# A fused attention and two-stage feed-forward kernel on one core: attention steps placed earlier in their slots, first moves joined, splits and last groups moved

## The chip, the cores and the metric

The kernel runs on one core of a Trainium2 chip. The metric is the device time of one execution in microseconds (us). Below, TensorE is the matrix engine (PE in the profile, PEld its weight loads), VectorE is DVE, the activation engine is ACT, GpSimd is POOL, and SyncE (SP) issues most of the DMAs. Each engine works through its own list of instructions in order and waits on semaphores that others raise.

## The reference

Three stages follow each other, all in float32.

```python
# 1. attention: B, H, S, D = 4, 8, 768, 48
for t in range(S):
    state = alpha[:, :, t, :, None] * state + einsum('bhd,bhe->bhde', k[:, :, t], v[:, :, t])
    y[:, :, t] = einsum('bhd,bhde->bhe', q[:, :, t], state)
# y becomes x of 3072 tokens by 384
# 2. four experts, each 384 -> 1024 -> 384
p = domain_probs / domain_probs.sum(-1)
out += p[:, e:e+1] * (maximum(x @ w1[e], 0) @ w2[e])
# 3. 384 -> 2048 -> 384
g = h - tanh(h)      # h = x @ w_in
result = g @ w_out
```

## The kernel before

Each float32 operand of a large product is kept as two rounded parts, a high one and the rest (low), and a product is three matmuls: high by high, high weights by low data, low weights by high data.

**Token sets and slots.** The 3072 tokens are six sets (m) of 512. A set has 48 slots: 32 of the experts (s, each 128 of the hidden columns) and 16 of the last stage (f). In expert slot s TensorE runs `first(m, s)` (L647, nine matmuls, x by w1), and then `second(m, s - 4)` (L661, nine matmuls, the hidden values by w2): LEAD is 4, so a second product comes four slots behind its first one. In slots 0 to 3 of the sets after the first it is instead `second2` (L683), the last four second products of the set before. The four seconds that are left follow slot 31. A group of second2 for one tile of 128 tokens is three matmuls of 384 columns.

**From a first product to its second one.** VectorE's `scale` (L1076) takes relu and the expert's probability; ACT's `hidden_high` (L859) makes the high part in HH; VectorE's `hidden_low` (L1089), one slot later, the rest in HL. HH has four places, so hidden_high of slot s first waits, by `wait_used` (L341), until the second product of slot s - 4 has read the place. That is the one that stands in the same slot s on TensorE.

**Attention units.** Attention works on 12 units (u) of 256 tokens. Units 0 and 1 are done ahead of the slots. Units 2m+2 and 2m+3 are done in the expert slots of set m, the even one from slot 0, the odd one from slot 16, in steps 0 to 16, one step a slot (`units_at`, L132); steps 1 to 16 for unit 2, whose step 0 is done ahead. Each engine has its part of a step (`attention` in each engine's program). On TensorE step 0 is `diagonal` (L523, 64 small matmuls), steps 1, 2, 4, 5, 7, 8 are `scores`, step 10 is `turn` (L560, eight transposes), step 11 `deltas` (L570) and step 14 `attend` (L587). The other steps are empty on TensorE. TensorE's step stands at the end of the slot, after the second product.

On ACT a slot is hidden_high first and then the step: step 9 `join` (five copies), step 10 `lay` (L775, eight copies of what turn wrote, into KJ), step 13 `carry_last` and `carry_own` (L787 and L803, eight copies of the states into VS), step 15 `high_x` (L818, the high part of the unit's x). deltas waits for all eight copies of lay, attend for all eight of the carries. On VectorE step 15 is `low_x` (L1045), and `diagonal` of the next unit waits for it (`bank_free`, L494: it takes the same two banks). `diagonal` of an even unit also waits until VectorE has read the last two hidden blocks of the set before. On GpSimd steps 3, 6 and 9 are `raise_keys` (L1290), which the scores of steps 4 and 7 and the turn of step 10 wait for, and step 13 is `prepare` (L1279), the tables and the first query rows of the unit after next.

**Weights of the first set.** They come from memory into four staging buffers (`stage`, L393, on SP), ACT makes the high part (`split_high`, L851), and VectorE or GpSimd the low part (`split_low`, L1139 and L1306). Weights 0 to 3, and 4 and 5, are split ahead of the slots, 6 and 7 in slots 0 and 1, and those from 8 on each four slots ahead of use. In the slots of the first set ACT's split_high stands behind hidden_high and the attention step, and GpSimd's split_low behind raise_keys.

**The x of a unit.** Rows of x that belong to the third block of 128 are kept aside in XS (unit 1: XSb) and moved by small DMAs into their places (`move`, L367, on SP; `move_half`, L832, on ACT). Unit 0 is moved by six DMAs on SP, unit 1 by three on SP and three on ACT. The first product of a set waits for them (`moved`).

**Start of the slots.** VectorE's list ends, ahead of slot 0, with carry_own(1), split_low(2), low_x(0), low_x(1), two copies of diagonal(2), split_low(3), rotate(2, 0), split_low(4), split_low(5). GpSimd's ends with split_low(0) and (1), a wait for the carries of unit 1, prepare(2), split_low(6) and (7).

**End.** The last four second products of the last set run by token tile: for each of the four tiles, f = 12, 13, 14, 15; then ACT copies the tile out and SP stores it.

Of the kernel before, what the change touches and what calls it, by code (L numbers as in the profile page):

```python
# [7 lines left out]
fp32 = mybir.dt.float32  # L8
f32r = mybir.dt.float32r
# [9 lines left out]
CH = 64  # L19
# [66 lines left out]
def own(u):  # L86

    return int(u == 1)
# [6 lines left out]
def turn_of(u):  # L95

    return len(same_set(u))
# [20 lines left out]
    return PG * (sum(states_in(v) for v in same_set(u)) + c)  # L118


def carried_at(u):
    return 8 * (turn_of(u) + 1)

# [8 lines left out]
def units_at(m, s):  # L132

    out = []
    for u, first in ((2 * m + 2, 0), (2 * m + 3, STAGGER)):
        if u < UNITS and (u == AHEAD) <= s - first < STEPS:
            out.append((u, s - first))
    return out


def program(nc, qka_d, v_d, dp_d, w1_d, w2_d, win_d, wout_d, mask_d, ones_d, ident_d, out_d):
    ctx = ExitStack()
    with ctx:
# [5 lines left out]
        def place(name, words, dt=fp32):  # L149
            offset[name] = at[0]  # L150
            at[0] += (4 * words + 31) // 32 * 32
            assert at[0] <= nc.sbuf_usable_end, name
            return nc.alloc_sbuf_tensor_at(name, [P, words], dt, offset=offset[name])
# [34 lines left out]
        TOT = [place("TOT", TOTALS), lend("TOTb", TOTALS, "XB1", 2 * KT * TB, UW)]  # L188
        T64 = [place(f"T64_{n}", CHUNKS) for n in range(2)]
        T64X = [place(f"T64X_{n}", CHUNKS // 2) for n in range(2)]  # L190
        XS = [place("XS", 2 * UT, f32r), place("XSb", 2 * UT, f32r)]

        scratch_d = nc.dram_tensor("scratch", (SLOTS, P, RW), fp32, kind="Internal").ap()
        probs_d = nc.dram_tensor("probs", (E * NTB * TT, P), fp32, kind="Internal").ap()
# [5 lines left out]
        def sem(name):  # L200
            return ctx.enter_context(nc.semaphore(name))
# [4 lines left out]
        def sems(name):  # L206
            return sem(name), sem(name + "_b")
# [16 lines left out]
        carried = sems("carried")  # L224
        x_high = sems("x_high")
        x_low = sems("x_low")
        moved = [sems(f"moved{j}") for j in range(KT)]

        prob_step = sem("prob_step")
        prob_turned = sem("prob_turned")  # L230
# [69 lines left out]
        def fill_bank(u, k):  # L300
            if u == AHEAD and k < 2:
                return h_bank[k]
            return bank[RING_ALONE * u + k % RING_ALONE] if u < AHEAD else a_bank[k % 2]
# [6 lines left out]

        def to_move(u, j, hh):

            src = XS[own(u)][CH * hh + SPARE * j:CH * hh + SPARE * (j + 1), :].rearrange("p (h t) -> p h t", h=2)
            dst = x_tile(u)[CH * hh + D:CH * hh + CH, :, j, x_tokens(u)]
            return dst.bitcast(fp32), src.bitcast(fp32)

        def state_slot(u, c):
            n = c if 0 < c < UC else (4 * (u % 2) if c == 0 else 4 * ((u + 1) % 2))
# [35 lines left out]
        def _(sp):  # L354
# [12 lines left out]
            def move(u):  # L367
                for j in (2, 0, 1):
                    sp.wait_ge(x_low[own(u)], 3 * turn_of(u) + (2 if j == 2 else 3))
                    for hh in range(1 if u == 1 else 2):  # L370
                        dst, src = to_move(u, j, hh)
                        sp.dma_start(dst, src).then_inc(moved[j][own(u)], 16)

            def attention(u, step):
                nxt = follower(u)
# [87 lines left out]
            probs(0)  # L463
            for g in range(2):
                stage(g + STAGES)
            move(0)
            move(1)
            for g in range(2, LEAD):
                stage(g + STAGES)
            attention(0, 15)  # L470
# [22 lines left out]
        def _(pe):  # L493
# [140 lines left out]
            def first_product(m, g, out, x_moved=False, x_mixed=False):  # L634
                order = (2, 0, 1) if x_moved else (0, 1, 2)
                for kt in order:
                    if x_moved:
                        for u in (2 * m, 2 * m + 1):
                            pe.wait_ge(moved[kt][own(u)], 32 * turn_of(u) + 32)
                    if x_mixed:  # L640
                        pe.wait_ge(x2_low, KT * m + kt + 1)
                    nc.tensor.matmul(out, w1(g, 0, kt), x_part(m, 0, kt), start=(kt == order[0]), stop=False)  # L642
                    nc.tensor.matmul(out, w1(g, 0, kt), x_part(m, 1, kt), start=False, stop=False)  # L643
                    last = nc.tensor.matmul(out, w1(g, 1, kt), x_part(m, 0, kt), start=False, stop=(kt == order[-1]))  # L644
                last.then_inc(hid, 1)
# [81 lines left out]
            for m in range(NTB):  # L727
                for s in range(SLOTS1):
                    first(m, s)
                    if s >= LEAD:  # L730
                        for kt in range(KT):
                            last = second(m, s - LEAD, kt)
                        last.then_inc(used, 1)
                    elif m:
                        second2(m - 1, SLOTS2 - LEAD + s)
                    for u, step in units_at(m, s):
                        attention(u, step)
                for kt in range(KT):
                    for s in range(SLOTS1 - LEAD, SLOTS1):
                        last = second(m, s, kt)  # L740
                        if kt == KT - 1 and s < SLOTS1 - 1:
                            last.then_inc(used, 1)
                    last.then_inc(mixed, 1)
                for f in range(SLOTS2):
                    first2(m, f)
                    if f >= LEAD:
                        second2(m, f - LEAD)
            for t in range(TT):
                for f in range(SLOTS2 - LEAD, SLOTS2):
                    second2(NTB - 1, f, [t])  # L750


# [1 line left out]
        def _(act):  # L754
# [63 lines left out]
            def high_x(u):  # L818
                x, t = x_tile(u), x_tokens(u)
                if u // 2 >= 2:  # L820
                    act.wait_ge(hid, SLOTS * (u // 2 - 1))
                act.wait_ge(filled[own(u)], filled_at(u, 18))
                if turn_of(u):
                    for j in range(KT):
                        act.wait_ge(moved[j][own(u)], 32 * turn_of(u))
                nc.scalar.activation(XS[own(u)][:, 0:UT], fill_bank(u, 18)[:, UT:2 * UT], ACT.Copy).then_inc(x_high[own(u)], 1)
                nc.scalar.activation(x[:, 0, 2, t], fill_bank(u, 18)[:, 0:UT], ACT.Copy).then_inc(x_high[own(u)], 1)
                act.wait_ge(filled[own(u)], filled_at(u, 19))
                nc.scalar.activation(x[:, 0, 0:2, t], fill_bank(u, 19)[:, :].rearrange("p (a t) -> p a t", a=2),
                                     ACT.Copy).then_inc(x_high[own(u)], 1)  # L830

            def move_half(u):  # L832
                for j in (2, 0, 1):
                    act.wait_ge(x_low[own(u)], 3 * turn_of(u) + (2 if j == 2 else 3))
                    dst, src = to_move(u, j, 1)
                    act.dma_start(dst, src).then_inc(moved[j][own(u)], 16)

            def attention(u, step):
                if step == 9:
# [74 lines left out]
            join(1)  # L914
            high_x(0)
            high_x(1)
            move_half(1)
            split_high(LEAD)
            split_high(LEAD + 1)
            for m in range(NTB):  # L920
# [22 lines left out]
        def _(dve):  # L943
# [101 lines left out]
            def low_x(u):  # L1045
                x, t = x_tile(u), x_tokens(u)
                dve.wait_ge(x_high[own(u)], 3 * turn_of(u) + 2)
                nc.vector.tensor_tensor(XS[own(u)][:, UT:2 * UT], fill_bank(u, 18)[:, UT:2 * UT], XS[own(u)][:, 0:UT].bitcast(fp32),
                                        ALU.subtract).then_inc(x_low[own(u)], 1)
                nc.vector.tensor_tensor(x[:, 1, 2, t], fill_bank(u, 18)[:, 0:UT], x[:, 0, 2, t].bitcast(fp32),  # L1050
                                        ALU.subtract).then_inc(x_low[own(u)], 1)
                dve.wait_ge(x_high[own(u)], 3 * turn_of(u) + 3)
                nc.vector.tensor_tensor(x[:, 1, 0:2, t], fill_bank(u, 19)[:, :].rearrange("p (a t) -> p a t", a=2),
                                        x[:, 0, 0:2, t].bitcast(fp32), ALU.subtract).then_inc(x_low[own(u)], 1)
# [173 lines left out]
            pick_diagonal(AHEAD, 1)  # L1228
            split_low(3)
            rotate(AHEAD, 0)  # L1230
            split_low(LEAD)
            split_low(LEAD + 1)
            for m in range(NTB):
                for s in range(SLOTS1):
                    scale(m, s)
# [17 lines left out]
        def _(pool):  # L1253
# [22 lines left out]
                pool.wait_ge(tabled[own(u)], 9 * turn_of(u) + 1)  # L1276
                distant(nc.gpsimd, u, 0).then_inc(spread[own(u)], 1)

            def prepare(u):  # L1279
                n = turn_of(u)  # L1280
                pool.wait_ge(a_in[own(u)], 16 * (n + 1))
                pool.wait_ge(rotated[own(u)], 3 * n)
                pool.wait_ge(keys_up[own(u)], 3 * n)
                pool.wait_ge(stated[own(u - 2)], stated_at(u - 2, states_in(u - 2)))
                tabulate(u, 0, 1)
                spread_queries(u)
                spread_distant(u)
                tabulate(u, 1, 9)

# [14 lines left out]
                    prepare(follower(u))  # L1304

            def split_low(g):  # L1306
                if g == LEAD + 2:
                    pool.wait_ge(w_low, g)
                pool.wait_ge(w_high, g + 1)
                nc.gpsimd.tensor_tensor(ring_split(g, 1), WS[g % STAGES][:, :].rearrange("p (w c) -> p w c", w=2),  # L1310
                                        ring_split(g, 0).bitcast(fp32), ALU.subtract).then_inc(w_low, 1)
# [9 lines left out]
            pool.wait_ge(prob_step, E + 2)  # L1321
            split_low(0)
            split_low(1)
            pool.wait_ge(carried[1], carried_at(1))
            prepare(2)
            split_low(LEAD + 2)
            split_low(LEAD + 3)
            for m in range(NTB):
                for s in range(SLOTS1):
                    for u, step in units_at(m, s):  # L1330
# [41 lines left out]
```

## Time and profile before

| what | value |
|---|---|
| median of three runs | 1385.35 us (1384.54 to 1385.61) |
| the profiled execution's own time | 1385.14 us |
| its span | 1383.3 us |
| TensorE busy | 1338.7 us, 97% |
| VectorE busy | 872.2 us, 63% |
| ACT busy | 573.6 us, 41% |
| GpSimd busy | 274.5 us, 20% |
| mean granted TensorE clock | 0.988 of full speed |

The span is from the first to the last instruction of one profiled execution; its own time is 1.8 us longer. Busy time counts instructions at work, not waits. A busy TensorE is not one at its peak, since matmuls overlap and their ends are modelled: with matmuls back to back, the distance between two starts (0.23 us for 512 columns, 0.17 us for 384) says what one costs, not its own duration.

### The profile page before, as it was taken

What the parts mean: (1) busy time and instruction counts of PE and PEld (TensorE: products, weight loads), DVE (VectorE), ACT (ScalarE), POOL (GpSimd) and SP (SyncE); (2) the same over time, 40 slices, a digit from 0 to 9 for tenths busy, and PEclk for the clock granted to TensorE, in tenths of its full rate; (3) what the DMA queues carried; (4) which work ended last, traced back from release to release, by engine and by line L of the source; (5) the groups of instructions that cost most, each with busy time, mean ns of one, the idle gap of its engine ahead of it and who ended that gap; (6) DMA issues with size and microseconds to landing.
All of it is one profiled execution on the core that took longest, in us unless ns stands there. A gap on an engine that the chain in (4) does not pass through costs nothing.

```text
span 1383.3 us, 25858 instructions
## 1 busy us (share of the span) xinstructions
PE 1338.7 (97%) x10177; PEld 1121.2 (81%) x10177; DVE 872.2 (63%) x1769; ACT 573.6 (41%) x1072; POOL 274.5 (20%) x272
## 2 busy tenths in 40 slices
PE   3599999999999999999999999999999999999998
PEld 3478788988878888878898887898887889888887
DVE  8884855994554875465687565497555478333395
ACT  1525346843214751414662323374231476211185
POOL 4566655004022001313001403000221000000000
PEclk8799999999999999999999999999999999999999
DMA  7389797856655656565655655665665465655551
GB/s 213 91 301 312 251 310 252 323 216 216 210 198 197 232 182 217 183 211 194 241 186 180 226 192 191 217 223 176 219 201 166 161 228 195 206 200 189 197 191 69
DMA packets 104968, 289.08 MB, mean 209 GB/s; under 512 B 10032, under 2 KB 64912, under 8 KB 104848
## 3 DMA queue, kind: packets, MB, share of 16 engines
q1 hardware_dynamic: 104704, 287.33, 61.8%
q8 instruction: 81, 1.33, 0.4%
q14 instruction: 39, 0.32, 0.1%
q10 hardware_dynamic: 144, 0.10, 0.0%
HBM read 242.52 MB, written 42.52 MB: 206 GB/s over the span
## 4 chain that ended last, share of the span: by engine, by line
PE 88%; DVE 6%; issue 3%; POOL 2%; ACT 1%; DMA 0%; DVEq 0%; POOLq 0%; ACTq 0%
PE bank L642 14%; PE bank L643 13%; PE bank L644 13%; PE bank L667 9%; PE bank L668 9%; PE bank L669 9%; PE bank L691 4%; PE bank L693 4%; PE bank L692 4%; PE bank L554 3%; PE bank L595 1%; DVE RG L1143 1%; PE bank L532 1%; DVE GG L1113 1%; DVE GG L1109 1%
## 5 line engine op out<-in xcount | busy, mean ns | idle before, releaser
L864 ACT ACTIVATE HH<-GG 128x512 fp32r<-128x512 f32 x192 | 121.2, 631 | 631.3 <-PE bank L669 507.3
L642 PE MATMUL bank<-XB,RG 128*128 128x512 f32 x864 | 349.3, 404 | 3.2 <-DMA XB<-XSb 2.8
L643 PE MATMUL bank<-XB,RG 128*128 128x512 f32 x864 | 340.1, 394 | 0.0
L644 PE MATMUL bank<-XB,RG 128*128 128x512 f32 x864 | 339.1, 392 | 0.0
L1086 DVE SCALAR_TENSOR_TENSOR GG<-bank,PB 128x512 f32<-128x512 f32 x192 | 133.3, 695 | 310.1 <-PE bank L644 309.9
L667 PE MATMUL bank<-HH,RG 128*128 128x512 f32 x576 | 224.3, 389 | 0.0
L668 PE MATMUL bank<-HH,RG 128*128 128x512 f32 x576 | 224.2, 389 | 0.0
L669 PE MATMUL bank<-HL,RG 128*128 128x512 f32 x576 | 224.0, 389 | 0.0
L1297 POOL TENSOR_TENSOR KU<-KU,TOT 128x256 f32<-128x256 f32 x88 | 68.8, 809 | 699.0 <-PE bank L554 699.0
L642 PEld LDWEIGHTS bank<-XB,RG 128*128 128x128 f32 x864 | 162.6, 188 | 44.1 <-issue 3.1
L644 PEld LDWEIGHTS bank<-XB,RG 128*128 128x128 f32 x864 | 162.6, 188 | 35.7
L643 PEld LDWEIGHTS bank<-XB,RG 128*128 128x128 f32 x864 | 162.8, 188 | 28.8
L1092 DVE TENSOR_TENSOR HL<-GG,HH 128x512 fp32r<-128x512 f32 x192 | 158.9, 827 | 8.9 <-ACT HH L864 8.8
L976 DVE COPY_PREDICATED SC<-masks,bank 128x192 f32<-128x192 int32 (+2 forms) x396 | 98.7, 356 | 68.7 <-PE bank L554 68.4
L691 PE MATMUL bank<-RG,HH 128*128 128x384 f32 x384 | 129.6, 337 | 1.5 <-DVE HL L1122 1.4
L693 PE MATMUL bank<-RG,HL 128*128 128x384 f32 x384 | 129.5, 337 | 0.0
L692 PE MATMUL bank<-RG,HH 128*128 128x384 f32 x384 | 128.9, 336 | 0.0
L667 PEld LDWEIGHTS bank<-HH,RG 128*128 128x128 f32 x576 | 108.1, 188 | 23.0
L669 PEld LDWEIGHTS bank<-HL,RG 128*128 128x128 f32 x576 | 108.1, 188 | 22.7
L668 PEld LDWEIGHTS bank<-HH,RG 128*128 128x128 f32 x576 | 108.1, 188 | 22.5
L1109 DVE TENSOR_TENSOR GG<-SQ,bank 128x512 f32<-128x512 f32 x96 | 65.7, 685 | 39.4 <-ACT TH L874 39.4
L873 ACT ACTIVATE SQ<-bank 128x512 f32<-128x512 f32 x96 | 57.2, 596 | 67.6 <-PE bank L644 67.6
(131 smaller groups left out, 1667.2 us busy)
## 6 DMA issues: line engine op xcount, KB each, us to landing
RG<-scratch SPq DMA_DIRECT2D x240, 768.0 KB, 4.3
scratch<-RG SPq DMA_DIRECT2D x48, 768.0 KB, 5.5
VS<-vp SPq DMA_DIRECT2D x11, 768.0 KB, 6.0
WS<-w SPq DMA_DIRECT2D x32, 192.0 KB, 3.5
PB<-probs SPq DMA_DIRECT2D x6, 1024.0 KB
AU<-qka SPq DMA_DIRECT2D x11, 512.0 KB, 5.3
R<-qka SPq DMA_DIRECT2D x11, 512.0 KB, 5.3
KU<-qka SPq DMA_DIRECT2D x11, 512.0 KB, 6.3
```

The source lines that it names most:

```text
L642: nc.tensor.matmul(out, w1(g, 0, kt), x_part(m, 0, kt), start=(kt == order[0]), stop=False)
L643: nc.tensor.matmul(out, w1(g, 0, kt), x_part(m, 1, kt), start=False, stop=False)
L644: last = nc.tensor.matmul(out, w1(g, 1, kt), x_part(m, 0, kt), start=False, stop=(kt == order[-1]))
L667: nc.tensor.matmul(out, w2(g, 0)[:, c], HH[:, h_slot(g)], start=(s == 0), stop=False)
L668: nc.tensor.matmul(out, w2(g, 1)[:, c], HH[:, h_slot(g)], start=False, stop=False)
L669: return nc.tensor.matmul(out, w2(g, 0)[:, c], HL[:, h_slot(g)], start=False, stop=(s == SLOTS1 - 1))
L691: nc.tensor.matmul(out, HH[:, h], w2(g, 0), start=(f == 0), stop=False)
L692: nc.tensor.matmul(out, HH[:, h], w2(g, 1), start=False, stop=False)
L693: last = nc.tensor.matmul(out, HL[:, h], w2(g, 0), start=False, stop=(f == SLOTS2 - 1))
L864: nc.scalar.activation(HH[:, h_slot(g)], GG[:, h_slot(g)], ACT.Copy).then_inc(high, 1)
L1086: nc.vector.scalar_tensor_tensor(GG[:, h_slot(g)], h_bank[s % 2][:, :], 0.0, PB[:, e * TB:e * TB + TB], op0=ALU.max, op1=ALU.mult).then_in ...
L1092: nc.vector.tensor_tensor(HL[:, h_slot(g)], GG[:, h_slot(g)], HH[:, h_slot(g)].bitcast(fp32), ALU.subtract).then_inc(low, 1)
```

## The change

1. **Slots.** On TensorE the attention step of an expert slot stands between the first and the second product, for all six sets. ACT's, VectorE's and GpSimd's order inside a slot is as before.
2. **Moves.** XS is one tile for both kinds of unit. Units 0 and 1 are moved together, three DMAs on SP and three on ACT, each of twice the size, once both units' parts are there. `moved` is one semaphore per block instead of two.
3. **Splits.** split_low(4) and (5) go from VectorE to GpSimd, ahead of (6) and (7).
4. **Tables of unit 2.** GpSimd's prepare(2) starts when rotate(1, 2) is done; the wait for the carries of unit 1 comes after its first table and spread_queries.
5. **Last groups.** Second products f = 12 and 13 of the last set run over all four tiles first, then 14 and 15 tile by tile.

```diff
@@ tables and addresses
+def moved_at(u):
+    return 32 * max(1, u)
-        XS = [place("XS", 2 * UT, f32r), place("XSb", 2 * UT, f32r)]
+        XS = place("XS", 2 * AHEAD * UT, f32r)
-        moved = [sems(f"moved{j}") for j in range(KT)]
+        moved = [sem(f"moved{j}") for j in range(KT)]
+        def to_move_first(j, hh):
+            src = XS[CH * hh + SPARE * j:CH * hh + SPARE * (j + 1), :].rearrange("p (h w) -> p h w", h=2)
+            dst = x_tile(0)[CH * hh + D:CH * hh + CH, :, j, :]
+            return dst.bitcast(fp32), src.bitcast(fp32)
@@ SP
+            def move_first():
+                for j in (2, 0, 1):
+                    for u in range(AHEAD):
+                        sp.wait_ge(x_low[u], 2 if j == 2 else 3)
+                    dst, src = to_move_first(j, 0)
+                    sp.dma_start(dst, src).then_inc(moved[j], 16)
-            move(0)
-            move(1)
+            move_first()
@@ TensorE
                     first(m, s)
+                    for u, step in units_at(m, s):
+                        attention(u, step)
                     if s >= LEAD:
                         for kt in range(KT):
                             last = second(m, s - LEAD, kt)
                         last.then_inc(used, 1)
                     elif m:
                         second2(m - 1, SLOTS2 - LEAD + s)
-                    for u, step in units_at(m, s):
-                        attention(u, step)
...
+            for f in range(SLOTS2 - LEAD, SLOTS2 - 2):
+                second2(NTB - 1, f)
             for t in range(TT):
-                for f in range(SLOTS2 - LEAD, SLOTS2):
+                for f in range(SLOTS2 - 2, SLOTS2):
                     second2(NTB - 1, f, [t])
@@ ACT
-            move_half(1)
+            move_first()
@@ VectorE
             rotate(AHEAD, 0)
-            split_low(LEAD)
-            split_low(LEAD + 1)
@@ GpSimd
                 tabulate(u, 0, 1)
                 spread_queries(u)
+                if pause:
+                    pool.wait_ge(carried[own(u - 1)], pause)
                 spread_distant(u)
                 tabulate(u, 1, 9)
...
-            pool.wait_ge(carried[1], carried_at(1))
-            prepare(2)
-            split_low(LEAD + 2)
-            split_low(LEAD + 3)
+            pool.wait_ge(rotated[1], 3)
+            prepare(2, carried_at(1))
+            for g in range(LEAD, RING):
+                split_low(g)
```

## Rows read from the trace of the kernel before

**Rows 1.** The page: the span, and busy time and instructions of each engine.
```profile
span 1383.3 us, 25858 instructions
PE 1338.7 (97%) x10177; PEld 1121.2 (81%) x10177; DVE 872.2 (63%) x1769; ACT 573.6 (41%) x1072; POOL 274.5 (20%) x272
```

**Rows 2.** Waits, whole span: engine, line, releaser: us in total, times, longest us.
```profile
ACT HH L864 <- PE bank L669: 507.3, 146, 5.6
```

**Rows 3.** Timeline of ACT, unit 5, slots 25 to 29: start us, us, instruction, [idle before].
```profile
415.23 1.29 ACT L773 ACTIVATE R<-SC 64x512 f32<-64x512 f32 x2
416.55 0.63 ACT L864 ACTIVATE HH<-GG 128x512 fp32r<-128x512 f32 x1
417.09 2.76 ACT L783 ACTIVATE KJ<-bank 64x192 f32<-64x192 f32 x8
...
430.48 0.63 ACT L864 ACTIVATE HH<-GG 128x512 fp32r<-128x512 f32 x1 [3.45 <-PE bank L669]
...
432.37 1.85 ACT L807 ACTIVATE VS<-ST 48x288 f32<-48x288 f32 x4
```

**Rows 4.** Timeline of PE, the same slots.
```profile
416.79 0.48 PE L642 MATMUL bank<-XB,RG 128*128 128x512 f32 x1
...
418.93 0.39 PE L667 MATMUL bank<-HH,RG 128*128 128x512 f32 x1
...
421.06 0.94 PE L581 MATMUL bank<-VS,KJ 64*48 64x48 f32 x64
...
430.22 0.39 PE L642 MATMUL bank<-XB,RG 128*128 128x512 f32 x1
...
432.26 0.39 PE L667 MATMUL bank<-HH,RG 128*128 128x512 f32 x1
```

**Rows 5.** Timelines of DVE and PE, from unit 2 to unit 3, slot 16.
```profile
142.20 0.68 DVE L1053 TENSOR_TENSOR XB<-bank,XB 128x512 fp32r<-128x512 f32 x1
```
```profile
141.96 0.39 PE L667 MATMUL bank<-HH,RG 128*128 128x512 f32 x1
...
144.09 0.40 PE L532 MATMUL bank<-R,KU 64*64 64x64 f32 x12
```

**Rows 6.** Timelines of DVE and PE, start of the second set, unit 4.
```profile
289.16 0.67 DVE L1110 TENSOR_TENSOR TH<-bank,TH 128x512 f32<-128x512 f32 x1
```
```profile
290.09 0.63 PE L532 MATMUL bank<-R,KU 64*64 64x64 f32 x27 [0.63 <-DVE TH L1110]
```

**Rows 7.** Timelines of POOL and PE, unit 3, raise_keys and scores of slot 20.
```profile
161.62 1.24 POOL L1297 TENSOR_TENSOR KU<-KU,AU 128x256 f32<-128x256 f32 x1
```
```profile
164.70 0.54 PE L554 MATMUL bank<-R,KU 64*64 64x96 f32 x13
```

**Rows 8.** Timelines of SP, PE and DVE, start of the slots.
```profile
66.83 2.01 SPq L372 DMA_DIRECT2D XB<-XSb  x3
```
```profile
69.09 0.76 PE L642 MATMUL bank<-XB,RG 128*128 128x512 f32 x1 [2.85 <-DMA XB<-XSb]
...
79.49 0.89 PE L554 MATMUL bank<-R,KU 64*64 64x96 f32 x32 [0.90 <-DVE SC L976]
```
```profile
69.15 0.40 DVE L995 COPY R<-R 128x256 f32<-128x256 f32 x1 [1.28 <-POOL TOT L1266]
...
73.60 1.92 DVE L1143 TENSOR_TENSOR RG<-WS,RG 128x768 fp32r<-128x768 f32 x2
```

**Rows 9.** Timeline of DVE, step 0 of unit 3, beside splits on POOL.
```profile
147.82 2.32 DVE L1000 TENSOR_TENSOR R<-R,AU 128x256 f32<-128x256 f32 x1
```

**Rows 10.** Busy time by stretch: stretch, length, PE, PEld, DVE, ACT, POOL, PE clock, DMA.
```profile
70.00:72.00 2.00, 2.00 (x6) 1.53 (x5) 2.00 (x3) 0.00 (x0) 1.84 (x3) 0.50 0.40 107
...
74.00:76.00 2.00, 2.00 (x38) 1.46 (x37) 2.00 (x3) 0.00 (x0) 0.70 (x1) 1.00 0.46 107
```

**Rows 11.** Timeline of PE, the last groups.
```profile
1372.65 0.44 PE L691 MATMUL bank<-RG,HH 128*128 128x384 f32 x1 [1.44 <-DVE HL L1122]
...
1380.18 0.34 PE L693 MATMUL bank<-RG,HL 128*128 128x384 f32 x1
```

More of the change, by code:

```diff
@@ L311, in to_move, with x_aside @@
         def to_move(u, j, hh):
-            src = XS[own(u)][CH * hh + SPARE * j:CH * hh + SPARE * (j + 1), :].rearrange("p (h t) -> p h t", h=2)
+            src = XS[CH * hh + SPARE * j:CH * hh + SPARE * (j + 1), :].rearrange("p (h w) -> p h w", h=2)[:, :, 0:UT]
             dst = x_tile(u)[CH * hh + D:CH * hh + CH, :, j, x_tokens(u)]
             return dst.bitcast(fp32), src.bitcast(fp32)
+        def to_move_first(j, hh):
+            src = XS[CH * hh + SPARE * j:CH * hh + SPARE * (j + 1), :].rearrange("p (h w) -> p h w", h=2)
+            dst = x_tile(0)[CH * hh + D:CH * hh + CH, :, j, :]
+            return dst.bitcast(fp32), src.bitcast(fp32)
+        def x_aside(u, part):
+            at = part * AHEAD * UT + own(u) * UT
+            return XS[:, at:at + UT]
         def state_slot(u, c):
@@ L369, in move @@
                     sp.wait_ge(x_low[own(u)], 3 * turn_of(u) + (2 if j == 2 else 3))
-                    for hh in range(1 if u == 1 else 2):
+                    for hh in range(2):
                         dst, src = to_move(u, j, hh)
-                        sp.dma_start(dst, src).then_inc(moved[j][own(u)], 16)
+                        sp.dma_start(dst, src).then_inc(moved[j], 16)
[4 more added lines that the diff above has]
+                    dst, src = to_move_first(j, 0)
+                    sp.dma_start(dst, src).then_inc(moved[j], 16)
             def attention(u, step):
@@ L637, in first_product @@
                     if x_moved:
-                        for u in (2 * m, 2 * m + 1):
-                            pe.wait_ge(moved[kt][own(u)], 32 * turn_of(u) + 32)
+                        pe.wait_ge(moved[kt], moved_at(2 * m + 1))
                     if x_mixed:
@@ L822, in high_x @@
                 act.wait_ge(filled[own(u)], filled_at(u, 18))
-                if turn_of(u):
+                if u >= AHEAD:
                     for j in range(KT):
-                        act.wait_ge(moved[j][own(u)], 32 * turn_of(u))
-                nc.scalar.activation(XS[own(u)][:, 0:UT], fill_bank(u, 18)[:, UT:2 * UT], ACT.Copy).then_inc(x_high[own(u)], 1)
+                        act.wait_ge(moved[j], moved_at(u - 1))
+                nc.scalar.activation(x_aside(u, 0), fill_bank(u, 18)[:, UT:2 * UT], ACT.Copy).then_inc(x_high[own(u)], 1)
                 nc.scalar.activation(x[:, 0, 2, t], fill_bank(u, 18)[:, 0:UT], ACT.Copy).then_inc(x_high[own(u)], 1)
@@ L830, in high_x, with move_first @@
                                      ACT.Copy).then_inc(x_high[own(u)], 1)
-            def move_half(u):
+            def move_first():
                 for j in (2, 0, 1):
-                    act.wait_ge(x_low[own(u)], 3 * turn_of(u) + (2 if j == 2 else 3))
-                    dst, src = to_move(u, j, 1)
-                    act.dma_start(dst, src).then_inc(moved[j][own(u)], 16)
+                    for u in range(AHEAD):
+                        act.wait_ge(x_low[u], 2 if j == 2 else 3)
+                    dst, src = to_move_first(j, 1)
+                    act.dma_start(dst, src).then_inc(moved[j], 16)
             def attention(u, step):
@@ L1047, in low_x @@
                 dve.wait_ge(x_high[own(u)], 3 * turn_of(u) + 2)
-                nc.vector.tensor_tensor(XS[own(u)][:, UT:2 * UT], fill_bank(u, 18)[:, UT:2 * UT], XS[own(u)][:, 0:UT].bitcast(fp32),
+                nc.vector.tensor_tensor(x_aside(u, 1), fill_bank(u, 18)[:, UT:2 * UT], x_aside(u, 0).bitcast(fp32),
                                         ALU.subtract).then_inc(x_low[own(u)], 1)
@@ L1277, in spread_distant, with prepare @@
                 distant(nc.gpsimd, u, 0).then_inc(spread[own(u)], 1)
-            def prepare(u):
+            def prepare(u, pause=0):
                 n = turn_of(u)
@@ L1306, in split_low @@
             def split_low(g):
-                if g == LEAD + 2:
+                if g == LEAD:
                     pool.wait_ge(w_low, g)
```

## The prediction

> **What bounds the kernel now.** I read the page first: TensorE is busy 97% of the span [rows 1], and by the timelines its matmuls stand shoulder to shoulder from 84 us to the end but for a few gaps of under 1.5 us. So nothing in the middle can be gained by removing a wait: there is none. A gain can come only from the start, where TensorE waits for moved rows and for VectorE [rows 8], and from the last four groups [rows 11]. A new wait of TensorE in the middle, on the other hand, costs its full length, and once for each attention unit.
>
> Next I read the waits. ACT's longest one is hidden_high waiting for a second product, 146 times, 507.3 us in all [rows 2]. That is the wait on the place in HH: hidden_high of a slot starts only when the second product of the same slot has ended. Harmless so far, but whatever ACT has to do for attention in that slot stands behind it. Now the second product is put behind TensorE's attention step. ACT's attention work is thus still released by the end of the slot's second product, while the TensorE step that needs it comes earlier by one second product, about 2.1 us. The question of each step is whether it had 2.1 us in hand.
>
> **The change part by part.** The stage read is unit 5; I write its slots by their steps. In what follows the slot's total is unchanged, so the end of each slot falls where it did.
>
> *deltas (step 11).* Before, the first product of step 11's slot starts at 416.79 and ends at 418.93, then comes the second, and deltas starts at 421.06 [rows 4]. ACT's join ends at 416.52, hidden_high starts at 416.55, and lay runs 417.09 to 419.85 [rows 3], which leaves TensorE 1.2 us in hand. After, deltas is wanted at 418.93. The slot of step 10 now ends with the second product, at 416.79. hidden_high starts 0.26 later, as it does at 430.48 after the second product that ends at 430.22 [rows 3, 4], so at 417.05. lay follows it by 0.54 and takes 2.76, so it ends at 420.35. TensorE waits 420.4 - 418.9 = 1.5 us. Ten units (2 to 11) have this: 15.0 us. Bounds: if lay kept its old place, 419.85 - 418.93 = 0.9 each; if join delays it by a further half copy, 2.0 each.
>
> *attend (step 14).* Before, the second product of step 13 ends at 430.22, hidden_high starts at 430.48, the two groups of carries follow and end at 432.37 + 1.85 = 434.22 [rows 3]; attend is after a second product that starts at 432.26 and takes 2.1, so it just fits. After, attend is wanted at 432.26, and nothing on ACT moves. Wait: 434.25 - 432.3 = 1.95, ten times, 19.5 us. Bounds 1.7 and 2.2 each; this is the surest term, as both ends are rows.
>
> *diagonal of the odd units (step 0).* Its banks are free when low_x of the unit before is done, 142.20 + 0.68 less some 0.05 of overlap, about 142.85 [rows 5]. It stood after a second product that starts at 141.96; now it is wanted at 141.96 itself. low_x follows high_x, which again follows hidden_high and so the second product of slot 15, whose end doesn't move. Wait 0.85, five units (3, 5, 7, 9, 11): 4.3 us. Bounds 0.5 and 1.1 each.
>
> *diagonal of unit 4.* At the second set VectorE is late, since it also splits weights in the stage before. diagonal already waited 0.63 for it, until 290.09 [rows 6]. Now it stands ahead of a second product of twelve matmuls (2.1 us), which no longer covers that wait: 2.7 us instead of 0.6. A later step got some 0.2 back from VectorE being just as late; I take 1.9, bounds 0 and 2.3. In later sets VectorE is ahead by then.
>
> *Scores behind raise_keys in the first set.* There GpSimd's split_low stands ahead of raise_keys and itself waits for ACT's split_high, which follows hidden_high, hence the second product. raise_keys of unit 3 ended at 161.62 + 1.24 = 162.86 and the scores that need it came at 164.70 [rows 7]: 1.8 in hand, and it now comes later against the wanted time by a second product plus scores, 2.9. So about 1.0 more, once. The other four such places in units 2 and 3 have 0.3 to 2.6 in hand by the same reckoning; bounds for all 0 and 4.
>
> *Start.* The first product waited for the first block of unit 1, whose DMAs SP issued at 66.83 behind the six of unit 0 [rows 8]. Now each queue issues one DMA for it as soon as low_x(1) allows, near 63; weight loads issued just before landed until 67.0 by ACT's wait for them, so I expect the first product near 67.2 instead of 69.09. VectorE's rotate(2, 0) waited 1.28 us for GpSimd's table [rows 8]; prepare(2) now has that table near 64.4, so this wait goes. The two splits, 1.92 us for both, leave VectorE's path. scale(0) then comes at about 72.3 instead of 75.4. Late next is the second hidden block: first product 1 ends near 73.4, scale(1) and hidden_low(0) end at 74.8, the picks take 1.9, and the scores that stood at 79.49 start at 76.85. Gain 2.6 us. On GpSimd the four splits end near 78.2 and raise_keys of unit 2 near 81.9, when its scores are wanted, so the moved splits cost nothing there, with no cover left. Bounds of the start's gain: 0 (GpSimd's splits and the table chain late) and 4.0 (all of 1.28 + 1.92 and a faster landing).
>
> The copies of rotate beside splits on GpSimd are a risk in this: in step 0 of unit 3 one took 2.32 us with splits running [rows 9]. The Trainium skill (SBUF — State Buffer, Who interferes with whom) says that a VectorE instruction with two SBUF inputs contends with a GpSimd instruction that reads SBUF. By that rule rotate(2, 0) would meet split_low(4) on GpSimd if it runs past 70 us. The row agrees in direction. It is inside the bounds above.
>
> *End.* Before, the third group of the last tile order waits 1.44 us for VectorE's HL of f = 14 and from 1372.65 to 1380.18 there are 41 starts [rows 11], 7.53 us where 41 by 0.1735 make 7.11. After, 24 more matmuls stand ahead of the first use of f = 14, 4.2 us instead of 1.0, so both waits go: 1.44 + 0.42 + 0.1 = 1.95. The tile stores come 1.0 us apart instead of 2.1; bounds 1.0 (the last store held up by the one before) and 2.2.
>
> **Sum.** 15.0 + 19.5 + 4.3 + 1.9 + 1.0 = 41.7 more, 2.6 + 1.95 = 4.55 less: 37.1 more. The profiled execution's own time was 1385.14, so 1422.2; the median of the runs shown is 0.2 higher, and I predict 1422.3. All low ends together (9 + 17 + 2.5 + 0 + 0 - 4 - 2.2 = 22) give 1407.5; all high ends (20 + 22 + 5.5 + 2.3 + 4 - 0 - 1 = 53) give 1438.
>
> **Rivals.**
> *A. The clock falls after the new waits.* Some 25 waits of 0.9 to 2.7 us appear. In the start, after two gaps of 2.6 and 2.85 us nearly in a row, the granted clock was 0.50, that is 1.2 GHz, for about 4 us, and back at 1.00 by 74 us [rows 10]. For it: those gaps are not much longer than the new ones. Against it: the gap of 1.44 us near the end left matmul distances at 0.17 [rows 11], and here dense work stands on both sides of every wait. Price: 4 us at half clock lose 2 us; if it struck at each of the 25, 50 us more, 1472. The Trainium skill (TensorE: Matmul & The Clock Gate, HAM oscillation) has idle stretches between bursts taking TensorE back to 1.2 GHz each time, which is this rival.
> *B. One of the two large waits doesn't appear*, because lay or the carries turn out to run earlier than I have them. For it: lay's old place was set by join and not by the second product. Against: the carries' chain is all rows. Price: 15 to 19 us less, about 1405.
> *C. Faster after all.* TensorE's waits stay hidden because ACT gets to its attention work before the slot's second product ends. Then only the start and the end count: 1385.14 - 4.55 = 1380.6. The place is hidden_high's wait; it would have to be released by an earlier second product than that of its own slot, which the 146 waits of [rows 2] speak against. It decides from the point where the new waits sum to under 4.6 us, 0.46 a unit.
> *D. The moves of the slots cancel the gains at the ends only*, near 1385: the new waits would be 0.46 a unit. No row gives that.
>
> **How the numbers follow.** Forecast 0.80, A 0.05, B 0.09, C 0.04, D 0.02. Range 1408 to 1432: the forecast's own terms rarely fall all on one side, and the low end takes in most of B. Two kernels of this length can be told apart from about 0.2%, 2.8 us. Faster 0.04, same 0.02, slower 0.94.
>
> **What would show it.** In the waits after: TensorE's deltas waiting for ACT's KJ copies, ten times near 1.5 us; attend waiting for ACT's VS copies, ten times near 1.95; diagonal waiting for low_x five times near 0.85 and for VectorE once near 2.7. TensorE's idle time from 84 us on should be about 43 us, up from under 4. The first product near 67.2, the scores of slot 2 near 76.9, and no gap over 0.3 us in the last groups. Wrong if hidden_high is seen to start before its slot's second product ends, or if matmul distances of 0.43 us follow the waits.

## The result and the profile after

The changed kernel takes 1429.22 us (median of five, 1427.06 to 1430.15) against 1385.1 before: ratio 1.0315, 95% interval 1.0304 to 1.0326. The prediction was 1422.3, in a range of 1408 to 1432. The profiled execution took 1428.65 us with a span of 1426.8, which is 43.5 longer than before [rows 1].

The page after, the same two lines as before:

```profile
span 1426.8 us, 25841 instructions
PE 1341.7 (94%) x10177; PEld 1122.8 (79%) x10177; DVE 872.2 (61%) x1767; ACT 573.8 (40%) x1072; POOL 282.7 (20%) x274
```

TensorE is busy for 3 us more and the span is 43.5 longer, so nearly all of the loss is new idle time. The waits from 84 us on say on whom (engine, line, releaser: us in all, times, longest). L602 is deltas, L616 attend, L553 diagonal, L575 the scores:

```profile
PE bank L616 <- issue: 17.9, 10, 1.9
PE bank L602 <- ACT KJ L805: 15.3, 10, 1.6
PE bank L553 <- DVE XB L1076: 4.5, 5, 0.9
PE bank L553 <- DVE TH L1133: 2.7, 1, 2.7
PE bank L575 <- DVE SC L999: 1.7, 2, 1.1
PE bank L575 <- POOL KU L1320: 1.1, 1, 1.1
PE bank L687 <- DVE HL L1115: 0.4, 1, 0.4
```

Together they are 43.6 us; before, the same stretch had 2.8. The counts are those of the units: ten, ten, five, one. The first row names no releaser, and the timeline has to be read for it. Here is ACT for unit 5, the stage of [rows 3]:

```profile
433.71 1.28 ACT L795 ACTIVATE R<-SC 64x512 f32<-64x512 f32 x2
435.62 0.63 ACT L887 ACTIVATE HH<-GG 128x512 fp32r<-128x512 f32 x1 [0.63 <-PE bank L689]
436.16 2.76 ACT L805 ACTIVATE KJ<-bank 64x192 f32<-64x192 f32 x8
...
450.52 0.63 ACT L887 ACTIVATE HH<-GG 128x512 fp32r<-128x512 f32 x1 [3.45 <-PE bank L689]
451.18 1.21 ACT L823 ACTIVATE VS<-ST 48x96 f32<-48x96 f32 x4
452.41 1.84 ACT L829 ACTIVATE VS<-ST 48x288 f32<-48x288 f32 x4
```

And TensorE beside it, as [rows 4]:

```profile
439.06 0.94 PE L602 MATMUL bank<-VS,KJ 64*48 64x48 f32 x64 [1.50 <-ACT KJ L805]
...
454.35 0.23 PE L616 MATMUL bank<-R,VS 128*48 128x64 f32 x1 [1.88 <-issue]
```

join ends at 434.99, and ACT then stands idle for 0.63 us, until the second product of the slot has ended; before, hidden_high followed join at once [rows 3]. lay ends at 438.92 and deltas starts at 439.06. The carries end at 452.41 + 1.84 = 454.25 and attend starts at 454.35: the wait that the profile lists without a releaser is the one for ACT's copies into VS.

What the waits cost is a little more than their length: between first product 5 and the last one they grew by 42.2 us, and the changed kernel fell back by 46.1 there, of which about 1.6 is a stretch at the lower clock (below). I took the start of every run of first products in both traces and followed by how much the changed kernel lags. First products are counted from 0; "start" is the lag at number 5. Each step of the lag is one term:

| term | predicted | measured in the lag |
|---|---|---|
| start, to first product 5 | -2.6 | -0.58 |
| deltas, ten | 15.0 | 16.4 |
| attend, ten | 19.5 | 20.1 |
| diagonal of odd units, five | 4.3 | 5.6 |
| diagonal of unit 4 | 1.9 | 3.7 |
| scores of unit 3 in the first set | 1.0 | 2.3 |
| end | -1.95 | -2.0 |
| small ones between | 0 | -2.0 |
| sum | 37.1 | 43.5 |

The small ones are mostly steps of -0.12 to -0.14 us just behind each deltas and attend, so these two cost somewhat less than their rows say.

The start, in the timelines of TensorE, GpSimd and VectorE after (compare [rows 8]):

```profile
66.40 0.47 PE L662 MATMUL bank<-XB,RG 128*128 128x512 f32 x1 [1.44 <-DMA XB<-XS]
...
74.94 0.89 PE L575 MATMUL bank<-R,KU 64*64 64x96 f32 x32 [0.99 <-DVE SC L999]
...
82.37 1.56 PE L575 MATMUL bank<-R,KU 64*64 64x96 f32 x32 [2.21 <-POOL KU L1320]
```
```profile
70.42 8.31 POOL L1333 TENSOR_TENSOR RG<-WS,RG 128x768 fp32r<-128x768 f32 x4
```
```profile
69.66 0.69 DVE L297 TENSOR_TENSOR R<-R,TOT 128x512 f32<-128x512 f32 x1
```

The scores of slot 2 start 4.55 us earlier than before (74.94 against 79.49), so the start won more than forecast at that point. Two slots later nearly all of it is given back: GpSimd's four splits run until 78.7, raise_keys stands behind them, and the scores that need it, now ahead of the second product, wait 2.21. At the end of that wait, and of the 2.73 us of unit 4, the granted clock fell to its lower level of 1.2 GHz; behind the waits of 1.9 us it did not. Stretch, length, busy times, granted clock (third number from the end):

```profile
82.40:86.40 4.00, 4.00 (x39) 3.29 (x40) 3.96 (x12) 0.00 (x0) 0.00 (x0) 0.58 1.04 392
...
300.40:304.40 4.00, 3.97 (x72) 3.88 (x73) 3.74 (x7) 0.63 (x1) 0.00 (x0) 0.57 0.02 4
...
454.00:458.00 4.00, 3.65 (x71) 3.30 (x72) 0.00 (x0) 0.25 (x1) 0.00 (x0) 1.00 0.04 13
```

The Trainium skill (TensorE: Matmul & The Clock Gate, HAM oscillation) describes idle gaps that send TensorE back to 1.2 GHz. This trace agrees for its two longest waits alone. The length of a wait doesn't settle it, though. All four profiles with unit 4's wait of 2.7 to 2.8 us (this one, e1, e3, e8) have the fall behind it, but in e3 a wait of 2.58 us had none:

```profile
156.11 0.89 PE L575 MATMUL bank<-R,KU 64*64 64x96 f32 x32 [2.58 <-DVE SC L999]
```
```profile
158.00:162.00 4.00, 4.00 (x19) 3.33 (x18) 1.89 (x7) 1.37 (x2) 1.19 (x1) 1.00 1.03 321
```

The start doesn't go this way in every run. The profile of e8, with the same lists up to here, looks the same. In those of e3, e4 and e9 the first split on GpSimd begins while rotate(2, 0) is still at work on VectorE; the last two instructions of rotate then take 2.0 to 2.3 us each, the scores of slot 2 start only at 78.23 in e4 and 78.07 in e9, and no wait over 0.3 us for raise_keys follows. At first product 5 the lead over the kernel before is 0.58 here, 0.96 in e8, and 0.80, 0.80 and 0.95 in those three. So these lists won less than 1 us at the start in either way.

### The profile page after: what moved, and what is told of

The parts are those of the page before. It is cut to its first block, busy times and chain, and to the rows that moved or that the text cites. A ratio compares the mean times of both kernels' runs of the same rounds, so it can differ in the third digit from the quotient of the medians.

```text
span 1426.8 us, 25841 instructions
## 1 busy us (share of the span) xinstructions
PE 1341.7 (94%) x10177; PEld 1122.8 (79%) x10177; DVE 872.2 (61%) x1767; ACT 573.8 (40%) x1072; POOL 282.7 (20%) x274
## 4 chain that ended last, share of the span: by engine, by line
PE 82%; DVE 8%; issue 5%; ACT 3%; POOL 3%; DMA 0%; DVEq 0%; ACTq 0%; POOLq 0%
PE bank L662 12%; PE bank L663 12%; PE bank L664 12%; PE bank L687 10%; PE bank L688 9%; PE bank L689 9%; PE bank L711 4%; PE bank L713 4%; PE bank L712 4%; PE bank L575 3%; ACT KJ L805 2%; PE bank L616 1%; DVE RG L1166 1%; PE bank L553 1%; DVE R L1023 1%
## 5 line engine op out<-in xcount | busy, mean ns | idle before, releaser
L662 PE MATMUL bank<-XB,RG 128*128 128x512 f32 x864 | 337.5, 391 | 1.8 <-DMA XB<-XS 1.4
L664 PE MATMUL bank<-XB,RG 128*128 128x512 f32 x864 | 338.0, 391 | 0.0
L663 PE MATMUL bank<-XB,RG 128*128 128x512 f32 x864 | 338.0, 391 | 0.0
L687 PE MATMUL bank<-HH,RG 128*128 128x512 f32 x576 | 234.6, 407 | 0.4 <-DVE HL L1115 0.4
L688 PE MATMUL bank<-HH,RG 128*128 128x512 f32 x576 | 225.7, 392 | 0.0
L1320 POOL TENSOR_TENSOR KU<-KU,TOT 128x256 f32<-128x256 f32 x88 | 74.2, 869 | 714.1 <-PE bank L575 714.1
```

Source lines behind the costliest of these rows:

```text
L687: nc.tensor.matmul(out, w2(g, 0)[:, c], HH[:, h_slot(g)], start=(s == 0), stop=False)
L688: nc.tensor.matmul(out, w2(g, 1)[:, c], HH[:, h_slot(g)], start=False, stop=False)
```

## The experiments

Ratios are against the kernel before, run beside each experiment on the same chip. T is the theory that ACT's attention work is held by hidden_high, which waits for the second product of its own slot.

### e1_order_alone: the kernel before with part 1 only

```diff
                     first(m, s)
+                    for u, step in units_at(m, s):
+                        attention(u, step)
                     if s >= LEAD:
...
-                    for u, step in units_at(m, s):
-                        attention(u, step)
```

> The kernel before with part 1 alone: TensorE's attention step stands between the first and the second product. Theory T (ACT's attention work is held by hidden_high, which waits for the second product of its own slot): the whole loss is here. Middle of the kernel +46 us as in the changed kernel, start +0.4 (raise_keys of unit 2 ended 0.4 us after first product 4), end 0: about 1431. Rival R (the loss comes from the parts around it, the splits moved to GpSimd, the joined moves or the shared semaphore): at most 1390 here.

Measured: 1431.89 us, ratio 1.0332 (1.0317 to 1.0348). The waits are those of the changed kernel again:

```profile
PE bank L595 <- issue: 17.9, 10, 1.9
PE bank L581 <- ACT KJ L783: 15.2, 10, 1.6
PE bank L532 <- DVE XB L1053: 4.5, 5, 0.9
PE bank L532 <- DVE TH L1110: 2.8, 1, 2.8
```

So the whole loss is in the order of TensorE's slots, and R falls. The lag grows by 46.1 us from first product 5 to the last one, in the changed kernel by 46.1 too.

### e2_order_back: the changed kernel with part 1 undone

```diff
                     first(m, s)
-                    for u, step in units_at(m, s):
-                        attention(u, step)
                     if s >= LEAD:
...
+                    for u, step in units_at(m, s):
+                        attention(u, step)
```

> The changed kernel with part 1 alone undone: attention step after the second product again, parts 2 to 5 kept. Theory T: no new waits in the middle. End -2.0. Start: the scores of slot 2 come 4.6 us earlier as in the changed kernel, and raise_keys of unit 2, which ends at 82.3 there, is wanted at about 82.1, so nearly all of it is kept: -4.3. Sum 1385.1 - 6.3 = 1378.8. Rival S (GpSimd's longer list takes back the start's gain in any order): -2.0 - 0.6, about 1382.5. Rival R: above 1400.

Measured: 1381.95 us (1378.51 to 1384.01, 11 runs), ratio 0.9974 (0.9966 to 0.9983). Faster than before, by 3.6 us. The new waits are gone; the start kept 1.5 us in the profiled run, not 4.3. S gave the nearer number, but not for its reason: TensorE waits for no GpSimd work here. In this profile rotate(2, 0) on VectorE is late. Its last two instructions, beside GpSimd's splits from 69.23 on:

```profile
69.79 2.14 DVE L297 TENSOR_TENSOR R<-R,TOT 128x512 f32<-128x512 f32 x1
71.86 2.06 DVE L301 TENSOR_TENSOR R<-R,TOT 128x256 f32<-128x256 f32 x1
```
```profile
69.23 4.40 POOL L1333 TENSOR_TENSOR RG<-WS,RG 128x768 fp32r<-128x768 f32 x2
```

In the changed kernel's profile the same two took 0.69 and 0.46 us, since the splits began only at 70.42. That is 3.05 us on the path of scale(0). It is no effect of putting the order back: e3, e4 and e9 have it too.

### e3_act_first: the changed kernel with ACT's slot turned round

```diff
-                    hidden_high(m, s)
                     for u, step in units_at(m, s):
                         attention(u, step)
+                    hidden_high(m, s)
```

> The changed kernel, with the two parts of an ACT slot exchanged: ACT's attention step first, hidden_high after it. TensorE's order stays as changed. Theory T: lay, the carries and high_x are no longer behind the wait for the second product, so TensorE's ten waits for deltas (16.4 us in all), ten for attend (20.1) and five for diagonal (5.6) go; unit 4's wait and those of the first set stay. 1429.2 - 42.1 = 1387.1. Rival R2 (these waits come from the length of the chain itself, or from banks, VectorE or GpSimd, not from ACT's order): within 5 us of 1429.

Measured: 1393.81 us, ratio 1.006 (1.0046 to 1.0074). TensorE's order is the slow one and 35.4 us are back. TensorE's waits from 84 us on:

```profile
PE bank L602 <- ACT KJ L805: 3.2, 2, 1.6
PE bank L575 <- DVE SC L999: 3.2, 2, 2.6
PE bank L553 <- DVE TH L1133: 2.8, 1, 2.8
PE bank L575 <- POOL KU L1320: 1.1, 1, 1.1
```

All ten waits for attend, all five for low_x and eight of the ten for deltas are gone, which shows T and refutes R2. The two that stay are in the first set, and they are why the time is 6.7 above what T gave. There ACT also splits weights, and join waits for rotate of step 9, so lay is late without any second product:

```profile
112.72 1.06 ACT L791 ACTIVATE QB<-R 64x1024 f32<-64x1024 f32 x1 [3.54 <-DVE R L1026]
113.81 1.29 ACT L795 ACTIVATE R<-SC 64x512 f32<-64x512 f32 x2
115.13 0.63 ACT L887 ACTIVATE HH<-GG 128x512 fp32r<-128x512 f32 x1
115.67 0.83 ACT L879 ACTIVATE RG<-WS 128x768 fp32r<-128x768 f32 x1
116.40 2.75 ACT L805 ACTIVATE KJ<-bank 64x192 f32<-64x192 f32 x8
```

Those two are worth 3.5 us of lag, one score wait of 2.6 in the first set some 1.4. Most of the remaining 1.8 is in the small steps, which are -0.4 in all here and -2.0 in the changed kernel: they came with the waits that are gone, and my 42.1 had left them out.

### e4_three_back: steps 0, 11 and 14 back behind the second product

```diff
                     for u, step in units_at(m, s):
-                        attention(u, step)
+                        if step not in (0, 11, 14):
+                            attention(u, step)
...
+                    for u, step in units_at(m, s):
+                        if step in (0, 11, 14):
+                            attention(u, step)
```

> The changed kernel, with TensorE's steps 0, 11 and 14 (diagonal, deltas, attend) put back behind the second product and the scores and turn left between the products. Theory T: only these three steps were short of time, so their waits go, and unit 4's wait with the half clock behind it (3.65) too: 1429.2 - 42.1 - 3.65 = 1383.5. What is left of the first set's waits behind raise_keys (2.3) and of the start's returned gain (4.1) stays. If the scores and the turn are short of time as well in all sets, above 1390.

Measured: 1391.55 us, ratio 1.0039 (1.0027 to 1.0052). Of the three steps' waits only unit 4's is left, at 0.7 us, as before the change. But the scores now wait for VectorE eight times, from 90 us on:

```profile
PE bank L575 <- DVE SC L1003: 4.8, 7, 2.8
PE bank L575 <- DVE SC L979: 1.2, 1, 1.2
PE bank L575 <- POOL KU L1324: 1.1, 1, 1.1
```

With diagonal at the end of its slot and the scores in the middle of the next ones, VectorE has one second product less between them for its picks and rotate. Most of this is in the first set: one wait of 2.77 us at 154.75, and behind it the granted clock was 0.5 for about 3 us, so the lag grows by 3.5 us there; in the third to the fifth set the scores wait only 0.2 us, once a set. That it is the shorter distance is argued from the order; no run lengthened it again. My expectation missed that: a distance between two steps shrinks also when only the later one moves.

### e5_last_groups: the kernel before with part 5 only

```diff
+            for f in range(SLOTS2 - LEAD, SLOTS2 - 2):
+                second2(NTB - 1, f)
             for t in range(TT):
-                for f in range(SLOTS2 - LEAD, SLOTS2):
+                for f in range(SLOTS2 - 2, SLOTS2):
```

> The kernel before with part 5 alone: second products 12 and 13 of the last set over all tiles first. Theory: the wait of 1.44 us for f = 14 and the slow restarts go, -2.0: about 1383.5 against 1385.5. Rival: the tile stores, now 1.04 us apart, hold the last one up, and nothing is gained: 1385.5.

Measured: 1383.2 us, ratio 0.9984 (0.9975 to 0.9993), 2.1 us less, as the theory had it. The profiled execution was the slowest of the eleven (1385.89): its start was 2.7 us late, its end 2.0 us shorter. No wait of TensorE is left in the last 20 us.

### e8_attend_back and e9_unit4_back: one step each put back

```diff
                     for u, step in units_at(m, s):
-                        attention(u, step)
+                        if not (step == 14):
+                            attention(u, step)
...
+                    for u, step in units_at(m, s):
+                        if step == 14:
+                            attention(u, step)
```

In e9 the condition is `(u, step) == (4, 0)`.

> The changed kernel with TensorE's step 14 (attend) alone put back behind the second product. Theory T: the ten waits for the carries go with their slow restarts, 20.1 us: 1429.2 - 20.1 = 1409.1. Rival: the carries end no earlier against the attend than that, because the waits of deltas shift them too; then part of the ten waits stays and the time is above 1415.

Measured: 1409.84 us, ratio 1.0176 (1.016 to 1.0191); 19.4 less than the changed kernel, 20.1 expected. All ten waits for attend are gone and the ten for deltas stay at 15.2 us in all, so the two are independent.

> The changed kernel with the diagonal of unit 4 alone put back behind its second product. It waited 2.73 us, and the granted clock was 0.50 for some 2.7 us behind it; the lag behind the kernel before grew by 3.67 there. Theory H (the half clock follows from that one wait): all 3.65 go, 1425.5. Theory W (only the wait's 2.1 go, the half clock comes from elsewhere, as from the late DMAs or the stage before): 1427.1, and the clock still falls near 300 us.

Measured: 1427.02 us, ratio 1.0301 (1.0287 to 1.0315). The time is W's and the clock is H's. Behind the place of the old wait the granted clock is now full:

```profile
300.40:304.40 4.00, 3.34 (x73) 2.53 (x72) 3.74 (x7) 1.26 (x2) 0.00 (x0) 1.00 0.58 201
```

So the fall came with that wait, whose going takes it away; the four profiles that have the wait all show the fall. The time came out at W's number because the scores of unit 4 now wait for VectorE (1.2 and 0.7 us) as in e4: the lag steps by 2.2 us there in place of 3.67 at the diagonal.

### e10_moves_alone: the kernel before with part 2 only

```diff
-            move(0)
-            move(1)
+            move_first()
```

with the joined XS, `to_move_first` and the single semaphores as in the change, on both queues.

> The kernel before with part 2 alone: the moves of units 0 and 1 joined. The first product starts near 66.5 instead of 69.1 us, but scale(0) stays behind rotate(2, 0) and two splits on VectorE and starts near 75.4, which sets the second picks and the scores at 79.5. Theory V (VectorE's path sets the start): at most 0.3 us gained, 1385.2. Rival M (the moves set it): 2.6 gained, 1382.9.

Measured: 1385.31 us, ratio 0.9999 (0.9991 to 1.0008). V's time, but by half for V's reason. TensorE in this run:

```profile
66.96 0.36 PE L553 MATMUL bank<-R,KU 64*64 64x64 f32 x1 [3.67 <-issue]
68.90 0.76 PE L662 MATMUL bank<-XB,RG 128*128 128x512 f32 x1 [1.57 <-DMA XB<-XS]
```

The first product didn't even start earlier: the joined moves, issued from 62.88 on, landed at 68.9. And the last small matmul ahead of it comes after a gap for which the profile names nothing. That gap was 2.58 us before, 0.93 after, 2.03 in e2, 3.67 here; the last section says what stands beside it in the traces.

### e6_splits_back and e11_splits_wait: where the splits belong

Both start from e2. e6 puts split_low(4) and (5) back on VectorE; e11 adds to GpSimd's list:

```diff
+            pool.wait_ge(queries_up[own(AHEAD)], 2 * turn_of(AHEAD) + 1)
             for g in range(LEAD, RING):
                 split_low(g)
```

> The kernel of e2 (order of the slots as before, parts 2 to 5 kept), with part 3 undone too: split_low(4) and (5) back on VectorE behind rotate(2, 0). Theory K: in e2's profile the last two copies of rotate(2, 0) took 2.14 and 2.06 us, where they took 0.69 and 0.46 in the changed kernel's, because splits ran on GpSimd beside them; moving the splits away thus gave 1.9 us and cost 3.05. With them back scale(0) starts near 72.8 instead of 73.84: 0 to 1 us faster than e2's 1382. Theory L (the splits are better on GpSimd): 1.9 slower than e2.

Measured: 1383.06 us (1380.3 to 1384.34), ratio 0.9979 (0.997 to 0.9988). The median is 1.1 us above e2's, where K had 0 to 1 less and L 1.9 more, and the intervals overlap: the runs don't tell the two kernels apart, and show no gain from moving the splits by themselves. In this profile rotate's last two took 0.69 and 0.42 us again, but the first product started only at 69.78, against 66.48 in e2's, so it doesn't show what the short rotate is worth.

> The kernel of e2 with one wait more on GpSimd: split_low(4) starts only when rotate(2, 0) has finished on VectorE. Theory K: rotate's copies take 0.69 and 0.46 us again, scale(0) starts near 71 instead of 73.84; the scores of slot 2 then follow the second picks at about 76.3 instead of 78: 1.5 to 3 us faster than e2, 1379 to 1380.5, and raise_keys of unit 2 (done near 82) is still in time for scores that stand behind a second product. Rival G (GpSimd's list becomes the bound, first products 4 and 5 wait for splits): as slow as e2 or slower.

Measured: 1380.63 us (1378.55 to 1384.16, 6 runs), ratio 0.9969 (0.9957 to 0.998), 4.6 us under the kernel before. rotate's last two take their short times, and the splits follow:

```profile
71.08 0.69 DVE L297 TENSOR_TENSOR R<-R,TOT 128x512 f32<-128x512 f32 x1
71.69 0.42 DVE L301 TENSOR_TENSOR R<-R,TOT 128x256 f32<-128x256 f32 x1
```
```profile
72.18 7.70 POOL L1333 TENSOR_TENSOR RG<-WS,RG 128x768 fp32r<-128x768 f32 x4 [3.04 <-DVE R L301]
```

K's mechanism is shown, in that rotate is short when no split runs beside it; G falls, since no first product waits for a split. K's price is not shown. The first product started at 68.55 here, 2.1 us later than in e2's profile, scale(0) waited for it, and the scores of slot 2 came at 78.34, no earlier than e2's 77.89. The medians differ by 1.3 us, inside the spread of both; e11 has the lowest median of all that I ran.

## Why the prediction was right, point by point

**The sum.** The forecast was 6.4 us of 43.5 too small, and the result lies 2.8 under the top of the range. The errors didn't cancel: every term of the middle was too small (41.7 forecast, 48.1 measured), the start's gain was too large, and only the small steps, which I had not foreseen, went the other way by 2.0.

**The bound.** That TensorE had no waits in the middle to lose, and that a new one would cost its full length once a unit, held: 46 us of lag come between first product 5 and the last one, and e1 has them alone.

**The mechanism.** That ACT's work for a step is released by the end of the slot's second product, while TensorE needs it one second product earlier, is shown by e3: with the same TensorE order and ACT's slot turned round, 23 of the 25 waits for ACT's work are gone.

**deltas and attend.** 1.5 and 1.95 a unit were forecast; for deltas the rows give 1.42 (420.35 - 418.93), which rounding made 1.5. Measured waits were 1.50 (1.63 in the first set) and 1.60 to 1.88, and the lag 1.6 and 1.8 to 2.1. For the two units of the first set the reason was only half right: join and a weight split alone make lay late (e3).

**diagonal.** 0.85 was forecast for odd units, the waits were 0.90 and the lag 1.12 each. The row for unit 4 had its wait right (2.73 against 2.7) and its price wrong: I credited 0.2 and left out the half clock behind it, 1.6 us more (3.67 of lag for 2.1 of added wait). Putting that step back gave less than that, as the scores behind it then wait (e9).

**The start** was mis-sized most: -2.6 forecast, -0.58 measured. The first half came out better (4.55 us at slot 2, in a run whose clock stayed at 1.00 there), but I wrote that raise_keys of unit 2 would be done just when wanted, with no cover left. With scale(0) earlier than I had it, the scores were wanted 2.2 us before raise_keys, which stands behind the splits, was done, and the clock fell behind that wait. In e3, e4 and e9 the gain was lost earlier, by the rotate beside splits that I had as a risk inside the bounds.

**The scores of the first set**: 1.0 forecast, 2.3 measured; the wait behind raise_keys was 1.14 as worked out, and two waits for VectorE's picks were not in the sum: one of 0.81 before grew to 1.15, one of 0.59 is new.

**The end**: -1.95 forecast, -2.0 in the trace and -2.1 by e5.

**The rivals.** A, the half clock behind every new wait, happened behind two, the longest of this run. B, C and D didn't happen; C's place, hidden_high's wait, was the right one to watch, since e3 removes it by another order.

## What to carry to other kernels

Before an instruction is moved ahead on the engine that bounds the kernel, list what it needs from each other engine and ask what releases that work: if it is the very instruction that was jumped over, as a buffer's reuse here, the wait is the length of the jump less what the step had in hand, in every iteration (here 0.9 to 1.9 us of a jump of 2.1). A step moved on one engine shortens the distance to the step before it as well, so a partial move needs the same check again (e4, e9). And parts that gain two or three microseconds are measured alone, or a loss of forty hides that they are worth having.

## What the runs showed of the hardware that I had not expected

- Two VectorE instructions with both inputs in SBUF took 2.14 and 2.06 us beside a GpSimd split, and 0.69 and 0.42 once the split waited for them. The Trainium skill (SBUF — State Buffer, Who interferes with whom) says that such an instruction contends with a GpSimd instruction that reads SBUF; e2 and e11 agree. It was in the prediction as a risk, not in its sum; the changed kernel's own profile doesn't have it, those of e3, e4 and e9 do.
- In the changed kernel waits of 2.21 and 2.73 us between dense matmuls were followed by a granted clock of 0.5 for about 3 us; the 25 waits of 0.9 to 1.9 us for ACT's and low_x's work were not. Nor was one of 2.58 us in e3, while one of 2.77 us at nearly the same place in e4 was. What decides between the last two is not shown.
- The start differs from run to run by up to 3 us with the same instructions. Ahead of one small matmul there is a gap for which the profile names no releaser: with the lists of the kernel before it was 2.58, 1.21 (e1) and 4.50 us (e5), with those of the change 0.93, 0.93 (e8) and 0.46 (e9). The scores of slot 2 came at 79.49, 79.81 and 82.18, and at 74.94, 74.61 and 78.07; the gap alone doesn't account for the last of these, where rotate was slow. The trace's list of DMA packets holds one of 16 KB on queue 8, of the kind "instruction", in that stretch. It ends at 64.48, 63.66, 66.19, 63.22, 62.98 and 64.08 us in these six, and the matmul starts 1.3 to 1.6 us behind it in all twelve profiles (in e4 the 63 matmuls ahead are not yet done then, and there is no gap). So TensorE most likely waits there for its next instructions; no experiment moved the packet, and why it comes earlier or later stays open.
